# Moving the last store of a token tile from SyncE's queue to an indirect DMA on GpSimd

## The reference, cut to what matters

```python
# 1. linear attention with a decayed state, per batch and head
y[:, :, t] = einsum('bhd,bhde->bhe', rt, state + (u * kt) x vt)
state = w * state + kt x vt
# 2. a dense layer with a leaky activation
h = x @ w_in; g = max(h, 0) + alpha * min(h, 0); x2 = g @ w_out
# 3. mixture of 8 experts, 384 tokens each
logits = x2 @ w_gate
# tokens are given to experts by descending logit, until each expert is full
h = maximum(x2[mask] @ w1[e], 0); out[mask] = h @ w2[e]
```

## Time and profile before

| | us |
|---|---|
| three executions | 803.66, 803.63, 805.52 (median 803.66) |
| the profiled execution's own time | 803.66 |
| its span in the profile | 801.9 |
| PE busy | 773.3 (96% of the span) |
| DVE busy | 499.9 (62%) |
| POOL busy | 474.1 (59%) |
| ACT busy | 219.8 (27%) |
| share of PE in the chain that ended last | 88% |
| share of DVE, of ACT and of DMA in it | 6%, 2%, 1% |

### The profile page before, as it was taken

One profiled execution on the slowest core, in us unless ns is written; L12 is line 12 of the kernel. 1 busy time (PEld: TensorE's weight loads), 2 busy tenths in 40 slices (PEclk: granted clock), 3 DMA queues, 4 the chain that ended last, 5 costly groups with the idle time before them and its releaser, 6 DMA issues.

```text
span 801.9 us, 16115 instructions
## 1 busy us (share of the span) xinstructions
PE 773.3 (96%) x6390; PEld 652.9 (81%) x6397; DVE 499.9 (62%) x1039; ACT 219.8 (27%) x453; POOL 474.1 (59%) x469
## 2 busy tenths in 40 slices
PE   6799999999999999999999999988999999999997
PEld 5578888888888888888888788756887988989996
DVE  8887766566655565666654344577777777776221
ACT  1233322111211121111112221204245244353451
POOL 6899985555555555555553332308377675775871
PEclk9999999999999999999999999989999999999999
DMA  8775522222222212222004000023532614507401
GB/s 227 222 198 154 150 71 69 69 66 73 60 65 65 62 61 68 70 69 67 14 11 168 11 31 1 10 91 128 188 109 108 217 41 178 187 32 268 166 13 48
DMA packets 47082, 78.34 MB, mean 98 GB/s; under 512 B 6304, under 2 KB 32032, under 8 KB 46624
## 3 DMA queue, kind: packets, MB, share of 16 engines
q1 hardware_dynamic: 38352, 59.42, 23.2%
q10 hardware_dynamic: 5584, 8.46, 3.7%
q0 software_dynamic: 3072, 9.44, 3.4%
HBM read 67.85 MB, written 9.44 MB: 96 GB/s over the span
## 4 chain that ended last, share of the span: by engine, by line
PE 88%; DVE 6%; ACT 2%; issue 1%; DMA 1%; POOL 1%; SPq 0%; POOLq 0%; DVEq 0%; ACTq 0%
PE bank L1396 24%; PE bank L1398 22%; PE bank L1397 22%; PE bank L1413 3%; PE bank L1447 3%; PE bank L1430 2%; PE bank L1506 2%; PE bank L1561 2%; PE bank L1663 2%; DVE both L921 1%; PE bank L1619 1%; PE bank L1466 1%; PE bank L1721 1%; PE bank L1711 1%; DMA raw<-w 1%
## 5 line engine op out<-in xcount | busy, mean ns | idle before, releaser
L538 POOL TENSOR_TENSOR gl<-g,gh 128x512 fp32r<-128x512 f32 x80 | 107.4, 1343 | 158.0 <-ACT gh L711 158.0
L1064 DVE TENSOR_SCALAR q<-bank,alpha_sb 128x512 f32<-128x512 f32 x96 | 71.9, 749 | 140.9 <-PE bank L1398 140.7
L711 ACT CAST gh<-g 128x512 fp32r<-128x512 f32 x80 | 49.7, 621 | 285.6 <-PE bank L1398 251.1
L1396 PE MATMUL bank<-xTh,win_h 128*128 128x512 f32 x288 | 113.4, 394 | 0.3 <-DVE xTl L957 0.3
L1398 PE MATMUL bank<-xTh,win_l 128*128 128x512 f32 x288 | 112.4, 390 | 0.0
L1397 PE MATMUL bank<-xTl,win_h 128*128 128x512 f32 x288 | 112.2, 390 | 0.0
L1396 PE MATMUL bank<-gh,wout_h 128*128 128x512 f32 x240 | 99.6, 415 | 1.1 <-DVE vs L948 0.5
L1398 PE MATMUL bank<-gh,wout_l 128*128 128x512 f32 x240 | 94.1, 392 | 0.0
L1397 PE MATMUL bank<-gl,wout_h 128*128 128x512 f32 x240 | 93.7, 390 | 0.0
L640 POOL TENSOR_TENSOR w1l<-raw,w1h 128x384 fp32r<-128x384 f32 x64 | 64.8, 1012 | 38.8 <-ACT w2h L792 37.9
L1396 PE MATMUL bank<-xeh,w1h 128*128 128x384 f32 x192 | 69.9, 364 | 0.0
(11 more groups left out here) (238 smaller groups left out, 1587.3 us busy)
## 6 DMA issues: line engine op xcount, KB each, us to landing
raw<-w SPq DMA_DIRECT2D x32, 768.0 KB
rt<-rT SPq DMA_DIRECT2D x48, 96.0 KB, 2.7
vs<-v SPq DMA_DIRECT2D x48, 96.0 KB, 2.8
vn<-v SPq DMA_DIRECT2D x24, 192.0 KB, 2.8
x2rows<-x2n SPq DMA_DIRECT2D x24, 192.0 KB, 1.9
kt<-kT SPq DMA_DIRECT2D x44, 96.0 KB, 2.5
kn<-kN SPq DMA_DIRECT2D x20, 192.0 KB, 2.4
rn<-rN SPq DMA_DIRECT2D x20, 192.0 KB, 2.6
```

The costliest lines, as they stand in the source:

```text
L538: nc.gpsimd.tensor_tensor(gl[:, f % 2], g[:, f % 2], gh[:, f % 2].bitcast(F32), ALU.subtract).then_inc(gl_ready, 1)
L711: nc.scalar.copy(gh[:, f % 2], g[:, f % 2]).then_inc(gh_ready, 1)
L1064: nc.vector.tensor_scalar(q[:, f % 2], h, 0.0, alpha_sb[:, f:f + 1], ALU.min, ALU.mult).then_inc(q_ready, 1)
L1396: nc.tensor.matmul(o, a_h, b_h, start=first, stop=False)
```

## The change

- SP no longer stores the last tile (chunk 5, batch 3).
- POOL gets a list of that tile's rows, `last_rows_at`, by an iota in the last chunk. Behind its last product split it waits for that list and for the last `x2n_ready`, and stores the tile by an indirect DMA with that list. It then waits for the stores of both buffers and for its own store, `last_stored`, and only then for `rows_marked`, behind which it forms `is_ar`. The waits for `x2_stored` ahead of `gather(0)` are gone; the one of buffer 1 counts one store less.
- PE's first `inverse` waits for the first tile of the last chunk (`KNOWN + 1`) and no longer for all 24.
- In SBUF, `wcol`, `pw`, `ipw` and `diag` lie ahead of `xTh`, and `lgT` lies behind `wc`, where it shares no bytes with later tiles.

```diff
--- before.py
+++ after.py
@@ -111,6 +111,10 @@
         kpow = sb("kpow", [P, H, HT], F32, one)
         knpow = sb("knpow", [P, DM], F32, one)
         u_sb = sb("u_sb", [P, DM], F32, one)
+        wcol = sb("wcol", [P, H], F32, one)
+        pw = sb("pw", [P, 7, H], F32, one)
+        ipw = sb("ipw", [P, 6, H], F32, one)
+        diag = sb("diag", [P, B, H], F32, one)
         xTh = sb("xTh", [P, 2, KD, TB], F32R, one)
         xTl = sb("xTl", [P, 2, KD, TB], F32R, one)
         x2T = sb("x2T", [P, KD, TB], F32, one)
@@ -120,10 +124,6 @@
         idle_b = sb("idle_b", [P, TB], BF16, one)
         down = q[:, 0].rearrange("p (h t) -> p h t", h=H)
         alpha_sb = sb("alpha_sb", [P, NF], F32, one)
-        wcol = sb("wcol", [P, H], F32, one)
-        pw = sb("pw", [P, 7, H], F32, one)
-        ipw = sb("ipw", [P, 6, H], F32, one)
-        diag = sb("diag", [P, B, H], F32, one)
         one.close()
 
 
@@ -134,16 +134,17 @@
         transposed.close()
         kept_h = sb("kept_h", [P, NF - 2 - KEPT, TB], F32R, ended)
         kept_l = sb("kept_l", [P, NF - 2 - KEPT, TB], F32R, ended)
-        lgT = sb("lgT", [P, TB], F32, ended)
-        sb("below_wcT", [P, KD * F - 2 * (NF - 2 - KEPT) * TB - TB], F32, ended)
+        sb("below_wcT", [P, KD * F - 2 * (NF - 2 - KEPT) * TB], F32, ended)
         wcT = sb("wcT", [P, TB], F32, ended)
         wc = sb("wc", [P, B, P], F32, ended)
+        lgT = sb("lgT", [P, TB], F32, ended)
         g_more = sb("g_more", [P, RING - 2, TB], F32, ended)
         pick = sb("pick", [P, E], F32, ended)
         ended.close()
 
 
         iota_b = sb("iota_b", [P, HALF], BF16)
+        last_rows_at = sb("last_rows_at", [P, 2], I32)
         beyond = sb("beyond", [P, NT, NS - 1])
         is_b = sb("is_b", [P, NT, HALF], FP16)
         is_a = sb("is_a", [P, NT, NS])
@@ -219,7 +220,7 @@
         gathered, xgt_done = [sem(f"gathered{a}") for a in range(NA)], sem("xgt_done")
         xgh_ready, xgl_ready = sem("xgh_ready"), sem("xgl_ready")
         early_ready, last_out = sem("early_ready"), sem("last_out")
-        rows_marked, rows_numbered = sem("rows_marked"), sem("rows_numbered")
+        rows_known, rows_marked, rows_numbered, last_stored = sem("rows_known"), sem("rows_marked"), sem("rows_numbered"), sem("last_stored")
         h2_done, g2h_ready, g2l_ready = sem("h2_done"), sem("g2h_ready"), sem("g2l_ready")
 
         load_begun, store_begun = sem("load_begun"), sem("store_begun")
@@ -435,7 +436,8 @@
                     load_next_heads(NCH - 1, 1)
             for c in range(NCH - 2, NCH):
                 for b in range(B):
-                    store(c, b)
+                    if (c, b) != (NCH - 1, B - 1):
+                        store(c, b)
 
             def load_expert(p):
 
@@ -613,6 +615,8 @@
                     nc.gpsimd.memset(grid[:], 0.0).then_inc(search_consts, 1)
                 if n == 4:
                     nc.gpsimd.iota(iota_b[:], [[1, HALF]], base=1, channel_multiplier=0, allow_small_or_imprecise_dtypes=True).then_inc(search_consts, 1)
+                if n == 3:
+                    nc.gpsimd.iota(last_rows_at[:], [[1, 2]], base=(NT - 1) * P, channel_multiplier=1).then_inc(rows_known, 1)
 
             for f in range(NF):
                 for n in (2 * f, 2 * f + 1):
@@ -620,6 +624,12 @@
                         search_const(n)
                 pool.wait_ge(gh_ready, NF * LAST + f + 1)
                 nc.gpsimd.tensor_tensor(gl_of(LAST, f), g_of(LAST, f), gh_of(LAST, f).bitcast(F32), ALU.subtract).then_inc(gl_ready, 1)
+            pool.wait_ge(rows_known, 1)
+            pool.wait_ge(x2n_ready, NT + OUT_PRE)
+            nc.gpsimd.indirect_dma_start(x2rows, bass.IndirectOffsetOnAxis(ap=last_rows_at[:, 0:1], axis=0), x2n[:, 1], None).then_inc(last_stored, 16)
+            for b in range(2):
+                pool.wait_ge(x2_stored[b], 16 * (NT // 2 + OUT_PRE - b))
+            pool.wait_ge(last_stored, 16)
             pool.wait_ge(rows_marked, 1)
             nc.gpsimd.tensor_tensor(is_ar[:], is_a[:], rowid[:].unsqueeze(2).to_broadcast([P, NT, NS]), ALU.mult).then_inc(rows_numbered, 1)
 
@@ -640,8 +650,6 @@
                     nc.gpsimd.tensor_tensor(w1l[:, f], raw1[:, p % 2, :, f * P:(f + 1) * P], w1h[:, f].bitcast(F32), ALU.subtract).then_inc(wlo1_ready, 1)
                     nc.gpsimd.tensor_tensor(w2l[:, f], raw2[:, p % 2, f, :], w2h[:, f].bitcast(F32), ALU.subtract).then_inc(wlo_ready, 1)
 
-            for b in range(2):
-                pool.wait_ge(x2_stored[b], 16 * (NT // 2 + OUT_PRE))
             gather(0)
             lo(0, range(NF2))
             for p in range(1, E):
@@ -1706,7 +1714,7 @@
                 pe.wait_ge(inverse_ready, 3 * p + 1 + half)
                 if p == 0 and half == 0:
                     pe.wait_ge(rows_numbered, 1)
-                    pe.wait_ge(x2n_ready, NT + OUT_PRE)
+                    pe.wait_ge(x2n_ready, KNOWN + 1 + OUT_PRE)
                 for j in range(half * NT // 2, (half + 1) * NT // 2):
                     mm = nc.tensor.matmul(banks[7][0:HALF, 0:NS], is_b[:, j], is_ar[:, j], start=(j == 0), stop=(j == NT - 1))
                 if half == 1:
```

## The result

The kernel after takes 810.85 us (median of 4, 810.71 to 811.81), the kernel before 804.28 us in the same series (4, 803.63 to 805.52). The ratio is 1.0083, 95% interval [1.0064, 1.01]: 6.6 us slower, where 0.9 us were forecast and 2.3 us were the upper end of the range. The profiled execution took 810.96 us, span 809.2.

A forecast was written before the change was run, and what follows sets the result against it. PE is full over most of the span, so the passage from dense layer to first expert (534 to 549 us) decides. The first product comes 0.9 us later: 803.66 + 0.9 = 804.6 us, range 803.2 to 806.0.

The forecast's parts named there:

- SP, one store less: SP's load of the expert's number and the weights behind it come earlier: bounds 0.5 and 0.9 us, 0.5 taken.
- POOL, the store's issue: POOL's indirect store begins 0.92 us after 534.71, at 535.63, paying a first indirect DMA's price that the gather is spared.
- Landing: POOL's store lands at 538.43 us, by the last scatter's 2.60 us plus 0.20 for the longer issue; bounds 536.9 and 542.2.
- B: Rival: weights started 0.5 us earlier stretch POOL's store by 1.3 us, 805.9 us; with the maximum +4.2, 807.9; chance 0.18.
- The inversion's length: PE's 24 matmuls ahead of idx keep their 1.67 us at half clock, ending at 540.72 instead of 539.44.
- The rule of the Trainium skill: In each DMA engine software and hardware queues take turns, so each store packet would wait for a weight packet once these flow.
- The added wait: POOL's wait for the landing ahead of is_ar makes the inversion, idx and DVE's chain come 1.3 us later.
- Where the chains meet: At xel, ahead of the first expert's product: routing decides, product at 549.95 against 549.04, +0.9 us; SP's gain worth nothing.
- C, the clock: Rival: PE's half clock lasts into the expert's first products, 0.17 us more each; 806.1 to 807.1 us; chance 0.04.
- Other edits: PE's weaker condition, the waits taken from the gather and the SBUF moves: all nothing.

The follow-up runs named there:

- e15: The kernel before with POOL's two waits for the stores ahead of is_ar instead of ahead of the first gather; ratio 1.0 to before.
- e3: The kernel after, but SP starts the first expert's weight loads only when GpSimd's store has landed; ratio 1.0078 to before.
- e2: The kernel before with an unused tile of 64 bytes ahead of xTh, nothing else moved; ratio 1.0034 to before.
- e10: The kernel before with an unused tile of 32 bytes behind xTl, so x2T, x2n and q move; ratio 1.0007 to before.
- e8: The kernel before with the last store issued from ACT's queue instead of SP's; ratio 0.9988, 802.80 against 803.58 us.
- e9: The kernel after with POOL's three waits for stores ahead of the first gather instead of is_ar; ratio 1.0063 to before.
- e1: The kernel before with only the change's SBUF moves; ratio 1.0035 to before.
- e16: The kernel after with an unused tile of 192 bytes ahead of xTh, 768 in all; ratio 1.0052 to before, 808.89 us.
- e11: The kernel before with 32 bytes ahead of g, so that g and all tiles behind it move together; ratio 0.9991 to before.
- e12: The kernel before with 32 bytes behind gl: g, gh and gl stay, the tiles behind them move; ratio 1.0032 to before.
- e17: The kernel before with the last store from ACT's queue and POOL's two store waits ahead of is_ar; ratio 0.9986, 803.46 against 804.36 us.

## Why the prediction was wrong, point by point

- **SP, one store less.** Right: weights issued 0.67 us earlier in relation to the copy, inside the bounds of 0.5 and 0.9.
- **POOL, the store's issue.** Right in its number, 537.87 - (536.50 + 0.48) = 0.89 us behind the copy, and 1.20 us long. Wrong in its reason, so the number was luck: e15 shows that 0.63 of the 0.92 us are no price of the first indirect DMA (0.29 us there); they went when the waits were taken from directly ahead of it. Only the 0.2 us longer issue belong to the first one.
- **Landing.** This step failed. I put 2.60 + 0.20 = 2.8 us, from a scatter with nothing beside it, and e3 measured just that for a store alone. Here the landing took 6.6 us, because the change itself had moved the weight DMAs to the same moment (issues at 537.87 and 538.00), and the store's first packet began 3.3 us later than without them (5.1 us behind its issue and 1.8 in e3). I had this as B, at 0.18, and argued against it that most of the store would be through when the weights flow densely. The trace of after shows not one of its packets up to 542 us. The maximum of the earlier trace rows, 6.4 us, was the row for this case; I gave it no place in the range. B's "+4.2 with the maximum" was right to 0.2 us, in part by luck: it adds 3.3 us to 2.8 us and so has a landing of 6.1 us, 0.5 too short, and the next step made up for some of it.
- **The inversion's length.** I kept the 1.67 us of before for PE's 24 matmuls and put them down to the half clock. In after they ran at half clock too, with everything ready, and took 1.41 us. The 1.67 us held a wait between the two halves, for the second half of `is_b` (the timelines of e2 and e10 list it as 0.32 us), so this term was 0.26 us too long:

```profile
545.20:546.60 1.40, 1.38 (x24) 1.38 (x26) 0.00 (x0) 1.38 (x4) 0.00 (x0) 0.50 0.05 12
```

- **The rule of the Trainium skill.** The Trainium skill, "DMA: Bandwidth & Descriptors", section "SWDGE vs HWDGE vs iDMA", has the two kinds of queues served in turn. By that rule a store whose descriptors are there would be held up by about the time of its own packets, which in e3 were through in about 1 us; that is an estimate. The trace does not show such a turn before 542 us: between 540 and 542 us the hardware queue moved 327 packets and GpSimd's none. Only from 543 us on do they share. Whether the store's descriptors arrive late, which would leave the rule untouched, or wait in line, no run here shows.
- **The added wait.** The chain behind it was right: the first product was to be late by the lateness of the inversion minus 0.4, and it was 0.5 less late than `idx` (`idx` 4.9 later in relation to the copy, the product 4.4). e15 adds that the wait costs nothing by itself.
- **Where the chains meet.** Right: `xel` has no wait for `xeh` ahead of it in after, and e8 shows the other side: without the store's delay SP's free queue is worth 0.4 us.
- **C, the clock.** Not in after, where it was back at the full level by 550 us, 5.7 us ahead of the product. In e9 it did fall to half once more, but ahead of the first product and not in it.
- **Other edits: "the SBUF moves change no instruction. All nothing".** This step failed too, and no rival held it. They cost 1.9 us in the stretch, because the matmuls that read `xTh` became 4 to 5 ns longer, and 0.0035 of the whole (e1, 2.8 us). Together, 2.8 and 4.4 us are 7.2 us, and the result's 6.6 us within its interval (5.1 to 8.0 us); e16 takes the one out and leaves 4.5.

## What to carry to other kernels

A DMA that is moved must be priced beside what is issued at its new time, by the slowest row seen under load, above all where the change itself brings its competitor forward. A wait is worth what it waits for: moved ahead of a whole engine's chain it is free at 1.9 us and costs 4.4 at 6.6. And a tile that moves in SBUF is an edit to every instruction that streams it: compare the mean of each group of matmuls by form ahead of the change's own place, before reading the place itself.

## What was not expected of the hardware

- Nine 512-column matmuls took 1.81 us from the first to the ninth start, or 1.87, with the same instructions, by the distance of the tile that they stream to other tiles: 0 bytes 1.81, 32 bytes 1.87, 64 and 576 about 1.84, 128 and 640 1.86, 256 and 768 1.81, 480 1.87 us. A period of 256 bytes fits all places tried, but only the places at 0, 256 and 768 test it; 64 and 576, 128 and 640 lie 512 apart. Moving everything from `g` on together changes next to nothing (e11). About half of it hangs on `g`, `gh` and `gl`, which VectorE, ScalarE, GpSimd and TensorE use at the same time (e12); that it is a conflict of such accesses is argued from this, not shown, and what the other half hangs on is open.
- A store of 128 rows from GpSimd's queue landed in 2.8 us alone and in 6.4 to 6.6 us when 1.5 MB of weights were issued from SyncE's queue at the same moment. Almost all of the difference is ahead of its first packet (1.8 us and 5.0 to 5.1 us behind the start of the issue), and for part of that time the engines were far from full (28.5% in 539.5 to 540 us of after). Why is open.
- An indirect DMA of GpSimd that stands directly behind several waits began 0.8 to 0.9 us after the last condition was met (the first gather in before 0.92 and in e9 0.8, the store in after 0.89), and 0.3 us when the earlier waits stood ahead of another instruction (after, e15, e17). `is_ar`, which is no DMA, began 0.2 us after the landing behind the same waits in after. Why is open.
